# Attention, a dense gated layer and a top-2 expert layer on one core: where GpSimd waits for its scatters, and where the last chunk and the router's matmuls stand

## What is computed

```python
x = attn(q, k, v)                      # 2 x 8 heads, 768 positions, width 64, local band of 96 + 8 global keys
x = x.reshape(1536, 512)
xn = x / sqrt(mean(x * x) + 1e-6) * rms_g
x = (silu(xn @ w_gate) * (xn @ w_val)) @ w_out          # dense layer, inner width 1536
logits = x @ w_gate2 + log1p(exp(x @ w_noise)) * noise  # router, 8 experts
top2 = two largest of each row; weights = softmax over the two
out[row] += weight * (relu(x[row] @ w1[e]) @ w2[e])     # for both experts e of a row, inner width 1024
```

## Time and profile before

| | us |
|---|---|
| median of 3 runs | 819.36 |
| lowest and highest run | 818.2, 823.47 |
| the profiled execution, whole | 821.36 |
| its span in the trace | 819.6 |
| TensorE busy | 776.6 (95%) |
| DVE busy | 380.9 (46%) |
| ACT busy | 321.6 (39%) |
| POOL busy | 208.5 (25%) |

### The profile page before, as it was taken

The page is one execution under the profiler, slowest core; times in us unless marked ns, Lnnn a source line. Parts: engine busy times, 40 slices in busy tenths (PEclk is TensorE's granted clock), DMA queues, the critical chain, the costliest instruction groups (busy, mean ns, idle before and its releaser), DMA issues.

```text
span 819.6 us, 11470 instructions
## 1 busy us (share of the span) xinstructions
PE 776.6 (95%) x4294; PEld 627.4 (77%) x4294; DVE 380.9 (46%) x716; ACT 321.6 (39%) x626; POOL 208.5 (25%) x280
## 2 busy tenths in 40 slices
PE   6999989999999999999999999899899998999893
PEld 4777657887778878788887887688788887888782
DVE  4777875542624235243254742453362535363321
ACT  4777864433242223331235422443242434342310
POOL 5467750000000300004000432232233323233230
PEclk9999999999999999999999999999999999999997
DMA  9868404410010000101134372445172555464320
GB/s 170 208 148 270 106 11 133 129 51 1 0 52 1 0 1 1 51 1 38 53 122 148 104 186 31 119 143 134 32 215 59 144 128 170 104 176 107 66 39 9
DMA packets 76298, 75.02 MB, mean 92 GB/s; under 512 B 46286, under 2 KB 53966, under 8 KB 76240
## 3 DMA queue, kind: packets, MB, share of 16 engines
q1 hardware_dynamic: 68560, 61.64, 26.5%
q0 software_dynamic: 7680, 12.62, 7.9%
HBM read 62.05 MB, written 13.75 MB: 92 GB/s over the span
## 4 chain that ended last, share of the span: by engine, by line
PE 65%; issue 16%; POOL 6%; DVE 4%; DMA 3%; ACT 3%; POOLq 1%; DVEq 0%; ACTq 0%
PE banks L512 25%; PE banks L542 12%; PE banks L1063 9%; PE banks L1042 4%; PE banks L1672 3%; DMA xT<-moe_rows,xT 3%; PE banks L1704 2%; POOL out_dram L949 2%; PE banks L1684 2%; PE banks L1644 2%; POOL xT L942 2%; PE banks L1668 1%; PE banks L1105 1%; PE banks L1019 1%; POOL scr L939 1%
## 5 line engine op out<-in xcount | busy, mean ns | idle before, releaser
L512 PE MATMUL banks<-XN,W_mid 128*128 128x512 f32 x552 | 135.3, 397 | 0.0
L512 PEld LDWEIGHTS banks<-XN,W_mid 128*128 128x128 f32 x552 | 103.5, 188 | 25.7 <-issue 1.0
L403 POOL DMA_INDIRECT slots<-entry,slot_x x24 | 23.9, 996 | 266.6 <-DVE slot_x L834 260.1
L1063 PE MATMUL banks<-W_mid,XN 128*128 128x512 f32 x240 | 72.9, 402 | 0.0
L512 PE MATMUL banks<-XN,W 128*128 128x512 f32 x288 | 70.5, 398 | 0.0
L512 PEld LDWEIGHTS banks<-XN,W 128*128 128x128 f32 x288 | 53.5, 188 | 14.4 <-issue 2.0
L1589 POOL TENSOR_TENSOR prob<-prob,rinv 128x512 f32<-128x512 f32 (+1 forms) x48 | 48.8, 1016 | 42.0 <-DVE rinv L1872 41.9
L753 DVE TENSOR_TENSOR act_b<-act_b,banks 128x512 f32<-128x512 f32 x36 | 24.7, 687 | 72.5 <-ACT act_b L641 69.4
L648 ACT ACTIVATE HT<-act_b 128x512 fp32r<-128x512 f32 x36 | 22.8, 632 | 90.2 <-DVE act_b L755 90.2
L1105 PE MATMUL banks<-W_mid,XN 128*128 128x512 f32 x180 | 57.0, 408 | 0.0
L641 ACT ACTIVATE act_b<-banks 128x512 f32<-128x512 f32 x36 | 21.5, 596 | 81.3 <-PE banks L512 81.2
(11 more groups left out here) (230 smaller groups left out, 1466.9 us busy)
## 6 DMA issues: line engine op xcount, KB each, us to landing
stage<-in_moe_w_dram SPq DMA_DIRECT2D x64, 512.0 KB, 3.7
rawv<-in_v_dram SPq DMA_DIRECT2D x16, 192.0 KB, 3.8
out_dram<-zrow SPq DMA_DIRECT2D x1, 3072.0 KB, 12.6
moe_rows<-xT SPq DMA_DIRECT2D x12, 256.0 KB, 2.5
rawq<-in_q_dram SPq DMA_DIRECT2D x14, 192.0 KB, 3.5
rawk<-in_k_dram SPq DMA_DIRECT2D x14, 192.0 KB, 4.4
stage<-in_moe_w_gate_dram SPq DMA_DIRECT2D x4, 512.0 KB, 4.1
stage<-in_moe_w_val_dram SPq DMA_DIRECT2D x4, 512.0 KB, 3.8
```

The costliest lines, as they stand in the source:

```text
L403: nc.gpsimd.indirect_dma_start(slots_d, bass.IndirectOffsetOnAxis(ap=slot_x[:, c * GT + t:c * GT + t + 1], axis=0), entry[:, c, t, :], Non ...
L512: last = nc.tensor.matmul(bank[2 * kind + n % 2][:], up_weight(kind, hw, k, c), xn[:, hx, k, :], start=(m == 0 and k == 0), stop=(m == 2 a ...
L1063: last = nc.tensor.matmul(bank[5 + t][:], he_pair[:, k, hh, t * P:(t + 1) * P], w2_part(e, hw, k), start=(q == 1), stop=(q == 24))
```

## The change

Five edits.

1. On POOL the scatter of a single tile is issued and not waited for. The wait for `sc1` stands where the scatter must have landed: in the loop ahead of the copies of this tile's index and gate, between experts ahead of `scatter_pair`, and at the end. In the loop the next tile's gather now comes first, with only its own index copied ahead of it. `free1` is gone; DVE waits for `sc1` itself. One gather into `y_one` ahead of the experts gives `sc1` its first count.
2. The turning of the first row tile of the next pair moves from (0, 8) to (0, 18), for experts 2 to 6.
3. At the change from expert 1 to expert 0 the first two weight pieces of expert 2 are split ahead of the single tile, not behind it, on ACT and DVE.
4. Dense layer: `up(11)` stands ahead of `down(9)`, and `down(9)`, `down(10)`, `down(11)` follow in a row. The sums of the logits of groups 0 and 1 go to bank 7, and the waits for `ez` and `lgr` stand ahead of the fourth quarter of `down(g, 0)` (which writes bank 7).
5. Last group: `turn_rows`, `logits`, `logits_sum`, `positions` stand behind up blocks 0, 2, 3 and 6 of expert 0. ACT takes `softplus` after its second hidden block.

```diff
         def logit_bank(g):
-            return bank[5 if g < NG - 1 else 6]
+            return bank[7 if g < NG - 1 else 6]
...
                     pe.wait_ge(sems["ytc"], GT * g)
-                    pe.wait_ge(sems["ez"], 2 * g - 1)
-                    pe.wait_ge(sems["lgr"], g)
                 for t in range(GT):
+                    if c == 0 and g >= 1 and t == GT - 1:
+                        pe.wait_ge(sems["ez"], 2 * g - 1)
+                        pe.wait_ge(sems["lgr"], g)
...
-                        else:
+                        elif c + 1 < FC - 1:
                             up(pe, g, c + 1)
+                        if c + 1 == FC - 2:
+                            up(pe, g, FC - 1)
...
-                else:
-                    turn_rows(g)
-                    logits(g)
-            pe_experts(pe, {0: lambda: logits_sum(NG - 1), 4: lambda: positions(NG - 1)})
+            pe_experts(pe, {0: lambda: turn_rows(NG - 1), 2: lambda: logits(NG - 1), 3: lambda: logits_sum(NG - 1),
+                            6: lambda: positions(NG - 1)})
...
             turned(NG - 1)
-            softplus(NG - 1)
-            act_experts(act, lambda: gate_exp(NG - 1))
+            act_experts(act, lambda: softplus(NG - 1), lambda: gate_exp(NG - 1))
...
                                              compute_op=ALU.add).then_inc(sems["sc1"], 16)
-                pool.wait_ge(sems["sc1"], (s + 1) * 16)
-                settle(c + 1).then_inc(sems["free1"], 1)
...
                     pool.wait_ge(sems["turn1"], one_turn(e, J))
+                    nc.gpsimd.tensor_tensor(idx[:, 1:2], lst[:, after, 0], zero_i[:], ALU.add).then_inc(sems["slot"], 1)
+                    pool.wait_ge(sems["slot"], one_count(e, J) * 3 - 2)
+                    settle(1)
+                    fetch_one(idx[:, 1:2])
+                    pool.wait_ge(sems["sc1"], (one_index(e, J) + 1) * 16)
                     nc.gpsimd.tensor_tensor(idx[:, 0:1], lst[:, here, 0], zero_i[:], ALU.add).then_inc(sems["slot"], 1)
                     nc.gpsimd.tensor_tensor(gate_t[:], lst[:, here, 1].bitcast(F32), scr[:, 0:1], ALU.add)\
                         .then_inc(sems["slot"], 1)
-                    nc.gpsimd.tensor_tensor(idx[:, 1:2], lst[:, after, 0], zero_i[:], ALU.add).then_inc(sems["slot"], 1)
                     pool.wait_ge(sems["slot"], one_count(e, J) * 3)
-                    settle(1)
-                    fetch_one(idx[:, 1:2])
                     scatter_one(idx[:, 0:1], one_index(e, J), 2)
...
+            pool.wait_ge(sems["y1"], 1)
+            nc.gpsimd.indirect_dma_start(y_one, None, xm[0:GN * (NG - 1), :],
...
+                pool.wait_ge(sems["sc1"], (before + 2) * 16)
+                settle(4)
                 scatter_pair(2 * e)
                 scatter_pair(2 * e + 1)
                 loop_one(e, n, before)
+            pool.wait_ge(sems["sc1"], (before + n) * 16)
+            settle(5)
...
-                    between |= {(0, 8): row(2 * e + 2), (1, 4): row(2 * e + 3)}
+                    between |= {(0, 18): row(2 * e + 2), (1, 4): row(2 * e + 3)}
...
                 dve.wait_ge(sems["l2e"], s + 1)
-                dve.wait_ge(sems["free1"], s + 1)
+                dve.wait_ge(sems["sc1"], (s + 1) * 16)
...
             n, before = tiles_of(act, 0)
+            act.wait_ge(sems["l2e"], before)
+            expert_high(act, 2, 0)
+            expert_high(act, 2, 1)
             one(before)
             pair_row_high(act, 4)
-            expert_high(act, 2, 0)
+            expert_high(act, 2, 2)
```

More of the change, by code:

```diff
@@ L277, in attention_moe_kernel @@
                 "ahead rowT0 rowT1 rowT2 turnT xbH xbL upT hbH hbL downT yT scT0 scT1 scT2 "
-                "row1 row_rest turn1 x1H x1L l1 rel1 th heH heL l2e y1 sc1 free1 slot ").split():
+                "row1 row_rest turn1 x1H x1L l1 rel1 th heH heL l2e y1 sc1 slot ").split():
             sems[name] = sem("m_" + name)
@@ L962, in loop_one @@
                         .then_inc(sems["slot"], 1)
-                    nc.gpsimd.tensor_tensor(idx[:, 1:2], lst[:, after, 0], zero_i[:], ALU.add).then_inc(sems["slot"], 1)
                     pool.wait_ge(sems["slot"], one_count(e, J) * 3)
-                    settle(1)
-                    fetch_one(idx[:, 1:2])
                     scatter_one(idx[:, 0:1], one_index(e, J), 2)
-            nc.gpsimd.memset(scr[:, 1:2], 0.0).then_inc(sems["free1"], 1)
             pool.wait_ge(sems["ahead"], 32)
             pool.wait_ge(sems["xm"], 16 * GT * (NG - 1))
+            pool.wait_ge(sems["y1"], 1)
+            nc.gpsimd.indirect_dma_start(y_one, None, xm[0:GN * (NG - 1), :],
+                                         bass.IndirectOffsetOnAxis(ap=pair_list(0)[:, 0:1], axis=0),
+                                         bounds_check=GN * (NG - 1) - 1, oob_is_err=False).then_inc(sems["sc1"], 16)
             for i in range(4):
@@ L1140, in pair_row_high, with act_experts @@
                                  row_bank(i).rearrange("p (c t) -> p c t", c=KC), ACT.Copy).then_inc(sems["xbH"], 1)
-        def act_experts(act, routing):
+        def act_experts(act, noise, routing):
             def one_row(x, xe=xe_one):
@@ L1170, in act_experts @@
                 pair_hidden(0, fb)
+                if fb == 1:
+                    noise()
                 if fb == 3:
@@ L1189, in act_experts @@
             n, before = tiles_of(act, 0)
+            act.wait_ge(sems["l2e"], before)
+            expert_high(act, 2, 0)
+            expert_high(act, 2, 1)
             one(before)
             pair_row_high(act, 4)
-            expert_high(act, 2, 0)
+            expert_high(act, 2, 2)
             pair_row_high(act, 5)
-            expert_high(act, 2, 1)
+            expert_high(act, 2, 3)
             one_row(before + 2)
-            expert_high(act, 2, 2)
-            expert_high(act, 2, 3)
             loop_one(0, n, before)
@@ L1292, in dve_experts @@
             n, before = tiles_of(dve, 0)
+            expert_low(dve, 2, 0)
+            expert_low(dve, 2, 1)
             one(before)
             pair_row_low(dve, 4)
-            expert_low(dve, 2, 0)
+            expert_low(dve, 2, 2)
             pair_row_low(dve, 5)
-            expert_low(dve, 2, 1)
+            expert_low(dve, 2, 3)
             one_row(before + 2)
-            expert_low(dve, 2, 2)
             one_out(before, lst[:, 2, 1:2].bitcast(F32))
-            expert_low(dve, 2, 3)
             loop_one(0, n, before)
```

## The result

| | before | after |
|---|---|---|
| median, us | 821.09 (4 runs, 818.2 to 823.47) | 797.5 (4 runs, 796.27 to 799.29) |
| ratio, 95% interval | | 0.9716 [0.9674, 0.9758] |
| profiled execution, its span | 821.36, 819.6 | 799.29, 797.5 |

The forecast was 799.7 (796 to 806), the likeliest of its cases. On a second chip the changed kernel had 798.39 against 823.03, a ratio of 0.9696 [0.9664, 0.9728].

The account below looks back on a forecast made before the run. TensorE, busy 95% of the span, was taken as the bound: its own work plus holes. Gains 16.6 + 1.4 + 2.1 - 0.4 = 19.7 us off a median of 819.36 gave 799.7 us, range 796 to 806.

Parts of the forecast that it names:

- Edits 1 and 2: Experts: nine TensorE holes for late gathers (7.5 and 5.3 us) close and two slow-clock stretches go, 16.6 us gained.
- Edit 3: Expert 0's single tile: TensorE's 1.2 us hole waiting for ACT goes, 1.4 us gained; bounds nothing to 1.4.
- Edit 4: Dense layer: holes of 0.27 and 0.60 us at each of two group changes go, 2.1 us gained.
- Edit 5: Hand-over to experts: 1.9 us of holes close, 2.3 open, a loss of 0.4; bounds gain 1.9 to loss 4.
- The hole at the ranking: Hand-over: the router's chain starts later, so TensorE waits at the ranking, a new hole of 0.8 us.
- The one at the turning of row tile 3: Hand-over: DVE delivers row tile 2's low part late, 11.4 us after counting picks, a new hole of 1.5 us.
- The doubt that the 3.2 us hole was an odd one: Experts: the longest pair hole may belong to this execution only, taking 2 to 3 us off the gain.
- Rival (a): Experts: gathers slowed by the scatter in front; if both slow by 2 us, 6 us more, 806 us; chance 0.10.
- Rival (b): Hand-over to the experts is dearer, losing 4 us instead of 0.4: 803 us; chance 0.14.
- (c): POOL: another wait holds it where sc1 did, so gathers go out no earlier: 816 us; chance 0.07.
- (d): Single tiles: scatter landing becomes the bound, costing beyond 9.6 us; slower, 828 us at a 12 us landing; chance 0.03.
- Settles: POOL: a settle may again meet DVE's two-operand subtraction and lose at most 1.1 us, covered by the gathers' room.

Follow-up runs that it names:

- no_e3: The changed kernel with expert 2's first two weight pieces split behind the single tile again: 799.41 us, against 798.39 for the changed kernel (6 runs each).
- pool_only: The kernel before with the POOL edit alone (scatter issued and not waited for, next gather first): 801.43 us, ratio 0.9729.
- hand_only: The kernel before with only the last group's reordering at the hand-over to the experts: 820.95 us (one run).
- dense_only: The kernel before with only the dense-layer edit (up(11) ahead of down(9), logits sums in bank 7): 819.02 us (one run).
- place_only: The kernel before with only the turning of a pair's first row tile moved from (0, 8) to (0, 18): 816.28 us (one run).
- no_pool: The changed kernel with the POOL edit undone, all other edits kept: 810.28 us, ratio 0.9842.

## Why the prediction was right

- *Edits 1 and 2, 16.6 us.* The changed kernel gains 18.7 between pair 1 and pair 7, with edit 3's 1.2 (`no_e3`) in it: 17.5. In `pool_only` it is 18.75 with 0.66 of the same hole in it (1.17 to 0.51): 18.1. So 0.9 to 1.5 more than forecast. All nine holes closed and the slow stretches went, as said. The place had no part in it: edit 1 alone does all of it.
- *Edit 3, 1.4 us.* 1.0 between medians, 1.16 to the last matmul.
- *Edit 4, 2.1 us.* 2.6 in the changed kernel, 2.4 alone.
- *Edit 5, a loss of 0.4.* A gain of 0.14. The term that was mis-sized is DVE's chain behind the count of picks. The hole at the ranking was worked out at 0.8 as a delay; it is 0.55 of printed idle, 0.71 with the 0.16, so that one is right. The one at the turning of row tile 3 was worked out at 1.5 and is 0.78, or 0.94 with the 0.16, because I took DVE's work from count to low part as 11.4 us without waiting. It took 461.39 - 450.45 = 10.9 us.
- *Sum.* 19.7 forecast; 21.4 in the stretches of the table, 22.1 in the two spans. Of the 2.4 us too few, 0.9 to 1.5 are in edits 1 and 2 and 0.5 each in edits 4 and 5; 0.7 lie ahead of the dense layer or behind the last matmul. The doubt that the 3.2 us hole was an odd one of its execution has no support: it or a sister of 3.6 and 3.9 us stands in `hand_only` and `dense_only` too. Between medians the gain is 821.09 - 797.5 = 23.6 us, 3.9 more than forecast. The forecast of 799.7 is only 2.2 off because it was counted from a median of 819.36, which one more run moved up to 821.09; that closeness is luck.
- *Rival (a).* The loops don't test it, since a second pass's gather brings no rows. Between experts the pair's gathers go out beside a scatter in flight. The trace of the changed kernel has only 10 of the 16 landings of L922, that of `pool_only` has all, so I compare that with before (the pair's gathers, before and `pool_only`):

```profile
DMA to landing us min/median/max: 3.3/4.0/5.7
```

```profile
DMA to landing us min/median/max: 3.6/4.6/5.9
```

The first gather behind the single tile's scatter is the one that must be in time. In the five experts it landed in 3.8, 3.6, 3.7, 5.7 and 3.7 us before, and in 5.4, 5.1, 4.7, 4.7 and 5.9 in `pool_only`, 1.4 more at the median. So (a) is likely real in kind: beside a scatter in flight a gather lands later. That the scatter is the cause was not tested apart, since the gather also goes out some us earlier among the weight loads. It costs nothing here, with 4.4 us to spare. The prediction's "never in flight together" held for the scatters of single tiles only; before, the loop's gather of 567.00 went out while the pair's scatter of 564.10 was in flight (landed 568.83), and landed in 2.8 us.

- *Rival (b)* fell with the two new holes at 1.3 us together, *(c)* with `pool_only`. *(d)* is far off: the scatter of 567.21 had landed by 572.41, 5.2 us, where it may take 9.6 by the prediction's count. No run made a scatter land late. In `pool_only`, all of them (L949):

```profile
DMA to landing us min/median/max: 4.5/5.0/6.0
```

- *Settles.* Some still take over 0.7 us (581.08, 0.74, between the rows of 579.59 and 583.35), and nothing waits for them, as said.

## What to carry to other kernels

When an engine that issues transfers in order waits for one of them to land, look at what is queued behind the wait. Here some 18 of the 21 us came from moving one wait behind the next gather's issue, with no matmul less. Then count a moved wait by all that stands behind it on every in-order engine: the gate's copy looked harmless by its own consumer, and 8.8 us more on it in each of eleven passes cost some 20 us, through DVE's queue. Look also at what the awaited transfer brings: four of the nine holes waited for gathers without rows. A hole that the new order opens can be worked out to about half a microsecond from a chain of rows, and closed by giving that chain's first step an earlier place.

## What I had not expected of the hardware

**The clock behind a hole.** The granted clock fell behind some holes of about 2 us and not behind others that were as long. Windows behind holes of 1.90 and 2.22 us in `place_only`:

```profile
583.50:587.00 3.50, 3.05 (x10) 2.57 (x11) 0.69 (x1) 1.66 (x2) 0.00 (x0) 0.60 0.00 0
760.50:764.00 3.50, 3.33 (x12) 2.75 (x13) 0.69 (x1) 1.66 (x2) 0.00 (x0) 0.67 0.00 0
```

and behind one of 2.13 us in `no_pool`:

```profile
581.50:585.00 3.50, 3.36 (x21) 3.00 (x22) 1.44 (x2) 1.66 (x2) 0.00 (x0) 1.00 0.00 0
```

It stayed up behind 2.15 us in `hand_only` too, and behind 2.10 in before. So the length of a hole doesn't decide it here, and what does is open. The fall costs 3.4 x (1 - 0.67) to 3.4 x (1 - 0.60), 1.1 to 1.4 us, so two kernels with nearly equal holes can differ by that much.

**Additions on POOL.** The same 24 one-column additions took 3.52 us in the loop and 6.01 between experts, 2.5 us more. DVE ran subtractions of weight pieces there, with two operands from SBUF, this one in the middle of them:

```profile
588.64 1.25 DVE L733 TENSOR_TENSOR W_mid<-stage,W 128x1024 fp32r<-128x1024 f32 x1 [0.19 <-ACT W L727]
```

The Trainium skill, GPSIMD Engine Reference, section Key points, says that GpSimd shares its SBUF interfaces with VectorE and contends with instructions that read two SBUF inputs; the trace agrees.
